# Dense layers in 512-token tiles, more unused products in the gap ahead of the experts, and one low half moved behind an expert's evictions

## What is computed

```python
y = attention_with_decaying_state(r, k, v, w, u)      # B=2, H=8, S=768, head_dim 48
x = y.reshape(1536, 384)
# mixture of 8 experts, one per token, capacity 384 per expert
logits = x @ w_gate; e = argmax(logits); g = softmax(logits)[e]
x = g * (relu(x @ w1[e]) @ w2[e])                     # w1: 384x1024, w2: 1024x384
# dense layers
h = x @ w_in                                          # 384 x 2048
out = (h - tanh(h)) @ w_out                           # 2048 x 384
```

## Time and profile before

| | us |
|---|---|
| median of 3 runs | 419.5 |
| the three runs | 415.28, 419.5, 419.82 |
| the profiled execution | 416.17 |
| its span, first to last instruction | 414.4 |
| TensorE busy | 392.7 (95%) |
| mean granted TensorE clock | 0.966 |

### The profile page before, as it was taken

One profiled execution on the slowest core, in us unless ns is written; L12 is line 12 of the kernel. 1 busy time (PEld: TensorE's weight loads), 2 busy tenths in 40 slices (PEclk: granted clock), 3 DMA queues, 4 the chain that ended last, 5 costly groups with the idle time before them and its releaser, 6 DMA issues.

```text
span 414.4 us, 10465 instructions
## 1 busy us (share of the span) xinstructions
PE 392.7 (95%) x3736; PEld 380.8 (92%) x3737; DVE 211.5 (51%) x453; ACT 182.5 (44%) x486; POOL 155.2 (37%) x132
## 2 busy tenths in 40 slices
PE   5999898999999999999999899999999999999991
PEld 4787777989999999999999899999999999999991
DVE  6365888655556455465455556524343434334340
ACT  5354456432666656657566354533132312231220
POOL 3564676604888815427246043352001100020002
PEclk9999999558999999999999999999999999999997
DMA  7488987443678585685776725101000100010001
GB/s 249 137 253 264 270 247 215 134 153 119 202 241 253 190 269 172 229 262 175 244 232 204 229 69 182 56 1 57 0 0 3 54 0 0 0 57 0 0 1 63
DMA packets 48454, 56.85 MB, mean 137 GB/s; under 512 B 3585, under 2 KB 46017, under 8 KB 48417
## 3 DMA queue, kind: packets, MB, share of 16 engines
q1 hardware_dynamic: 35936, 46.23, 35.5%
q10 hardware_dynamic: 10512, 5.31, 4.5%
q0 software_dynamic: 1968, 4.83, 3.1%
HBM read 46.23 MB, written 10.13 MB: 136 GB/s over the span
## 4 chain that ended last, share of the span: by engine, by line
PE 89%; DVE 5%; issue 2%; DMA 1%; ACT 1%; POOL 0%; POOLq 0%; SPq 0%; DVEq 0%; ACTq 0%
PE ring L1065 13%; PE ring L1067 13%; PE ring L1066 13%; PE pO L1317 8%; PE pO L1316 8%; PE pO L1065 5%; PE pO L1067 5%; PE pO L1066 5%; PE pY L1189 3%; PE pA L1140 2%; PE pD L1094 2%; PE ring L1205 2%; PE pY L1174 1%; PE ring L1254 1%; DVE kw L784 1%
## 5 line engine op out<-in xcount | busy, mean ns | idle before, releaser
L459 POOL TENSOR_TENSOR w_lo<-raw_weights,w_hi 128x768 fp32r<-128x768 f32 x40 | 73.7, 1845 | 85.1 <-ACT w_hi L580 84.9
L1007 DVE SCALAR_TENSOR_TENSOR minus_tanh<-square,ring 128x384 f32<-128x384 f32 x64 | 35.5, 554 | 93.3 <-ACT square L730 93.3
L580 ACT ACTIVATE w_hi<-raw_weights 128x768 fp32r<-128x768 f32 x80 | 67.1, 846 | 24.3 <-DMA raw_weights<-w 24.2
L730 ACT ACTIVATE square<-ring 128x384 f32<-128x384 f32 x64 | 31.5, 491 | 94.3 <-DVE h_hi L1017 53.8
L1065 PE MATMUL ring<-yT_hi,w_hi 128*128 x192 | 65.0, 338 | 1.7 <-DVEq L1002 1.7
L1067 PE MATMUL ring<-yT_hi,w_lo 128*128 x192 | 64.9, 338 | 0.0
L1316 PE MATMUL pO<-w_hi,h_hi 128*128 128x384 f32 x192 | 64.9, 338 | 0.0
L1317 PE MATMUL pO<-w_lo,h_hi 128*128 128x384 f32 x192 | 64.8, 338 | 0.0
L1066 PE MATMUL ring<-yT_lo,w_hi 128*128 x192 | 64.8, 338 | 0.0
L1065 PE MATMUL pO<-h_hi,w_hi 128*128 128x224 f32 x192 | 53.3, 278 | 0.0
L550 POOL DMA_INDIRECT out<-out_rows,tok x12 | 11.7, 974 | 111.1 <-ACT out_rows L725 107.2
(11 more groups left out here) (158 smaller groups left out, 762.3 us busy)
## 6 DMA issues: line engine op xcount, KB each, us to landing
raw_weights<-w SPq DMA_DIRECT2D x80, 384.0 KB, 4.0
x_by_slot<-x ACTq DMA_DIRECT2D x9, 576.0 KB, 5.8
x_expert<-x_by_slot SPq DMA_DIRECT2D x8, 576.0 KB, 5.6
kv<-kv_by_token SPq DMA_DIRECT2D x22, 192.0 KB, 4.3
rkT<-rk_by_feature SPq DMA_DIRECT2D x18, 192.0 KB, 3.8
rkT<-rk_by_feature SPq DMA_DIRECT2D x3, 512.0 KB, 5.3
x_expert<-x_by_slot SPq DMA_DIRECT2D x1, 384.0 KB, 3.0
x_by_slot<-x,sloti POOLq DMA_INDIRECT x12, 4.6
```

The source lines that it names most:

```text
L459: pool.tensor_tensor(lo, unit_raw(2, k), hi.bitcast(F32), ALU.subtract).then_inc(w2_ready, 1)
L580: act.activation(hi, unit_raw(what, k), ACT.Copy).then_inc(w1_hi if what == 1 else w2_hi, 1)
L730: act.activation(sq[:, i % 2, :], ring[i % 4][:, 0:CAP], ACT.Square, scale=THIRD ** 0.5, accum_out=sqsum[:, bass.ds(t * (2 * FC) + i, 1)]) ...
L1007: dve.scalar_tensor_tensor(out=nt[:, i % 2, :], in0=sq[:, i % 2, :], scalar=1.0, in1=ring[i % 4][:, 0:CAP], op0=ALU.subtract, op1=ALU.mult ...
```

## The change

Three things, and what they need of memory:

1. The dense layers go in three tiles of `TD` = 512 tokens instead of four of 384. `ring`'s matmuls stream 512 columns, the second layer has four blocks k and so four banks `pO`. The fourth takes the bank of `pF`; the flag's product goes to `ring[0]`. `ost` has more rows and takes the room of `xTh` and `xTl`, which the dense layers do not need.
2. In the gap, `keep_warm(3)` is new ahead of the last `logits`, `keep_warm(2)` becomes `keep_warm(8)`, and the six products `direct(10)` and `direct(11)` go ahead of the wait for `xe_in` and of `loaded`. `ring_full` is now signalled by `loaded`.
3. On VectorE, `low(e + 1, 3)` goes from ahead of `second` to behind it.

```diff
+TD = 4 * P
+TN = N // TD
...
+        exp = ExitStack()
+        xTh = sb("xT_hi", [P, KD, CAP], F32R, exp)
+        xTl = sb("xT_lo", [P, KD, CAP], F32R, exp)
+        exp.close()
+        ost = sb("out_rows", [P, 2 * KD, D], F32)
+        hh = sb("h_hi", [P, FC, TD], F32R)
...
-        pO = [ctx.enter_context(nc.psum_tensor(f"pO{i}", [P, 512], F32)) for i in range(3)]
-        pF = ctx.enter_context(nc.psum_tensor("pF", [P, 512], F32))
+        pO = [ctx.enter_context(nc.psum_tensor(f"pO{i}", [P, 512], F32)) for i in range(TD // P)]
...
-                    for k in range(4):
+                    for k in range(3):
                         low(e + 1, k, 1 - s)
                     by_width(dve, own, lambda cols: second(j, s, cols))
+                    low(e + 1, 3, 1 - s)
...
             near, far = slice(0, NARROW), slice(NARROW, CAP)
+            keep_warm(3, ones[:, :], pA[:, 0, 0, :])
             logits(STEPS - 1)
...
             direct(9, 2, near, False, False)
-            keep_warm(2, ones[:, :], pX[:, 0:P])
+            keep_warm(8, ones[:, :], pX[:, 0:P])
+            for c in range(KD):
+                direct(10, c, near, False, False)
+                direct(11, c, near, False, False)
             pe.wait_ge(xe_in, 16)
             for c in range(KD):
                 loaded(c, 0, slice(0, P))
-                loaded(c, 1, slice(0, NARROW - P))
-            for c in range(KD):
-                direct(10, c, near, False, False)
-                direct(11, c, near, False, True).then_inc(ring_full, 1)
+                loaded(c, 1, slice(0, NARROW - P)).then_inc(ring_full, 1)
...
+                width = CAP if general else TD
+                blocks = width // P
+                y = bass.ds(t * width, width)
...
-                            last = split_product(ring[i % 4][:, 0:CAP], W1h[:, s, c, f * P:(f + 1) * P],
+                            last = split_product(ring[i % 4][:, 0:width], W1h[:, s, c, f * P:(f + 1) * P],
...
-                    order = [(f, k) for f in range(streamed) for k in range(3)]
-                    order += [(f, k) for k in range(3) for f in range(streamed, FC)]
+                    order = [(f, k) for f in range(streamed) for k in range(blocks)]
+                    order += [(f, k) for k in range(blocks) for f in range(streamed, FC)]
...
-            with pe.Fori(0, TC) as t:
-                dense(t, E * RING + KD, ring_full, ring_done, o_full, o_done, False)
+            with pe.Fori(0, TN) as t:
+                dense(t, E * RING + KD, ring_full, ring_done, o_full, False)
             pe.wait_ge(flag_in, 1)
-            pe.matmul(pF[:, 0:1], ones[:, :], allok[:, :], start=True, stop=True).then_inc(flag_full, 1)
+            pe.matmul(ring[0][:, 0:1], ones[:, :], allok[:, :], start=True, stop=True).then_inc(flag_full, 1)
```

More of the change, by code:

```diff
@@ L261, in build @@
         o_done = sem("o_done")
-        o_sc = [sem(f"o_scattered{i}") for i in range(3)]
+        o_sc = [sem(f"o_scattered{i}") for i in range(TD // P)]
         tok3_made = sem("tok3_made")
@@ L543, in rows_out @@
             def rows_out(done, scattered, t, made):
-                pool.tensor_copy(tok3[:, :], tok_i[:, bass.ds(t * 3, 3)]).then_inc(made, 1)
+                m = len(scattered)
+                pool.tensor_copy(tok3[:, 0:m], tok_i[:, bass.ds(t * m, m)]).then_inc(made, 1)
                 pool.wait_ge(made, t + 1)
-                for i in range(3):
-                    pool.wait_ge(done, t * 3 + (i + 1))
+                for i in range(m):
+                    pool.wait_ge(done, t * m + (i + 1))
                     pool.sem_inc(passed, 1)
@@ L554, in landed @@
             def landed(scattered, t):
-                for i in range(3):
+                for i in range(len(scattered)):
                     pool.wait_ge(scattered[i], t * 16 + 16)
-            with pool.Fori(0, TC - 1) as t:
+            with pool.Fori(0, TN - 1) as t:
                 rows_out(o_done, o_sc, t, tok3_made)
@@ L718, in _, with rows @@
                     by_width(act, own, lambda cols: second(j, s, cols))
-            def rows(full, done, free, t):
-                for i in range(3):
-                    act.wait_ge(full, t * 3 + (i + 1))
+            def rows(full, done, free, t, m):
+                for i in range(m):
+                    act.wait_ge(full, t * m + (i + 1))
                     if i == 0:
@@ L739, in _ @@
                         high(1, E + 1, k, 1)
-            rows(o_full, o_done, ost_free, 0)
-            with act.Fori(1, TC) as t:
+            rows(o_full, o_done, ost_free, 0, TD // P)
+            with act.Fori(1, TN) as t:
                 for i in range(2 * FC):
                     squares(t, i)
-                rows(o_full, o_done, ost_free, t)
+                rows(o_full, o_done, ost_free, t, TD // P)
             act.wait_ge(flag_ready, 1)
@@ L748, in _ @@
             with act.If(large > 0):
-                for i in range(3):
-                    act.wait_ge(o_sc[i], TC * 16)
+                for i in range(TD // P):
+                    act.wait_ge(o_sc[i], TN * 16)
                 with act.Fori(0, TC) as t:
@@ L1210, in loaded @@
                 at = slice(k * P + cols.start, k * P + cols.stop)
-                pe.matmul(ring[c][:, at], xe[:, k, c * P:(c + 1) * P], ident[:, cols], start=False, stop=False,
-                          skip_group_check=True)
+                return pe.matmul(ring[c][:, at], xe[:, k, c * P:(c + 1) * P], ident[:, cols], start=False, stop=True,
+                                 skip_group_check=True)
             near, far = slice(0, NARROW), slice(NARROW, CAP)
+            keep_warm(3, ones[:, :], pA[:, 0, 0, :])
             logits(STEPS - 1)
@@ L1295, in _, with dense @@
                     by_width(pe, own, lambda cols: second(j, s, cols))
-            def dense(t, base, full, done, o_full, o_done, general):
-                y = bass.ds(t * CAP, CAP)
+            def dense(t, base, full, done, o_full, general):
+                width = CAP if general else TD
+                blocks = width // P
+                y = bass.ds(t * width, width)
                 for s in range(2):
@@ L1347, in _ @@
                 with pe.Fori(0, TC) as t:
-                    dense(t, 0, g_ring_full, g_ring_done, g_o_full, g_o_done, True)
+                    dense(t, 0, g_ring_full, g_ring_done, g_o_full, True)
 def kernel(r, k, v, w, u, moe_w_gate, moe_w1, moe_w2, moe_capacity, moe2_w_in, moe2_w_out):
```

49 lines of the change are left out of this document (22 added, 27 removed).

## The result

| | before | changed |
|---|---|---|
| median of 4 runs, us | 417.39 (415.22 to 419.82) | 421.81 (418.95 to 424.26) |
| the profiled execution, us | 416.17 | 421.67 |
| its span, us | 414.4 | 419.8 |
| mean granted clock in it | 0.966 | 0.962 |

The ratio is 1.019, with a 95% interval of 1.012 to 1.026: in this measurement, of four executions each, the changed kernel was 1.9% slower. The forecast was 419.1 us and no difference; 421.8 lies just outside its range.

A forecast was written before the change was run, and what follows sets the result against it. The prediction took TensorE as the bound: matmul count, spacing, its few stands, and half clock in the gap. Terms -2.9 (tiles) + 0.9 (low half) + 1.6 (gap) = -0.4 us gave 419.1 us on the median; range 413.0 to 421.5.

The forecast's parts named there:

- From there on TensorE never stands up to 98.65: Gap: after three unused products push `logits` by 0.62 us, all later work moves by 0.62; whole gap term +1.6 us.
- Rival E: Gap: the fill costs more than the dense layers give, up to +3.2 us; total +1.2, time 420.7; chance 0.24.
- rise at 95.85: Gap: the clock rises from half speed at 95.85 as in the trace before, giving the +1.6 us term.
- rival B: Gap: the fill lifts the clock early, gap term 0; total -2.0 us, time 417.5; chance 0.14.
- 512 columns, -2.9 us: Dense layers: 432 `ring` matmuls at 228 ns, 98.5 us, replace 576 at 176 ns, 101.4 us; -2.9 us.
- The line through two widths: Dense layers: a straight line through 224 columns (111 ns) and 384 (176 ns) gives 228 ns for 512.
- rival C: Dense layers: time on top of the columns vanishes, 213.3 ns per matmul, -9.2 us; total -6.7, time 412.8; chance 0.05.
- The moved low half, +0.9 us: End of the last expert: the low half delays the signal TensorE awaits before the dense layers; +0.9 us, bounds 0 and +1.0.
- the same 0.96 us stands between the evictions and the signal: Last expert, VectorE: the moved low half's 0.96 us comes before signal `y_ready`, for which TensorE waits; taken as +0.9 us.
- The lower bound, 0: End of the last expert: least cost allowed for the moved low half, 0 against the +0.9 us taken.
- The base: Whole kernel: difference set against 419.5 us, median of three timed runs; the profiled execution took 416.17 us.
- the bound of 0 for the 512-column matmuls: Dense layers: keeping the 384-column rate per column, 234.7 ns per matmul, the wider tiles gain exactly 0.

The follow-up runs named there:

- p3_gap_back: Kernel before plus fill and reorder, with nine products taken out of a body not entered, so later code is unmoved; ratio 1.001, median 0.0 us against before.
- e1_tiles: Kernel before with the 512-token dense tiles alone, gap and VectorE's order as before; ratio 0.998, median -0.9 us against before.
- p2_after_back: Changed kernel with nine products taken out of a body not entered, moving later code back; ratio 0.996, median -3.5 us against before.
- f2_no_fill: Changed kernel without the nine additional unused products; tiles, reorder and moved low half stay; ratio 0.995, median -2.6 us against before.
- e2_gap: Kernel before with the gap's part alone, nine more unused products and the reorder; ratio 1.007, median +5.9 us against before.
- g2_no_fill_pad: f2_no_fill plus nine unused products in a body not entered, so later code moves; ratio 1.012, median +4.7 us against before.
- f3_pad4: Kernel before with four unused products in a body not entered, so only later code moves; ratio 0.999, median +3.0 us against before.
- f1_changed: The changed kernel run again on another chip, with twelve executions; ratio 0.999, median +3.3 us against before.
- p1_pad: Kernel before with nine unused products in a body not entered, so only later code moves; ratio 1.012, median +5.2 us against before.

## Why the prediction was wrong

**The sum left out the code itself.** For part 2 I counted each added product's time and each wait, and "From there on TensorE never stands up to 98.65" was carried on to the first expert: the 0.28 us of "issue" at 100.06 was taken as a constant. This step failed: it is the end of a jump, it was 0.28 to 1.41 us in kernels with unmoved code, and it became 1.75 to 3.5 us in the kernels with the code moved by nine products, with a second stand of 1.5 to 2.6 us in the second expert in all of them but the first profile of the changed kernel (there the transfer had landed at 127.34, ahead of the transposes at 128.27, while in the other four it began behind their start; why it came early is open). The prediction had no term for where the code stands, and no rival with one.

Rival E had the right sign and the right place, but its price was the fill's execution. That price is there, but hardly counts. p3_gap_back and e1_tiles both spend 3.4 us of the gap at half clock. From the start of the last `logits` to the last unused products it is 96.40 - 85.27 = 11.13 us with the fill, and 93.02 - 83.24 = 9.78 without, so the fill takes TensorE 1.35 us in this pair of profiles. But the first expert's matmul comes 12.63 and 12.26 us behind `logits`, only 0.37 us apart, since e1_tiles then stands 1.34 us and p3_gap_back 0.36. In the whole kernel the fill's execution is lost in the noise: p3_gap_back is at 0.0 us by the median, with a ratio interval worth -1.8 to +2.8 us, and p2_after_back against f2_no_fill, on two chips, is at -3.5 and -2.6.

**The clock.** I let it rise at 95.85 as in the trace of before. In the changed kernel's profile it was up by 92, as rival B had it, but kernels with the old gap had it up by then too (in e1_tiles four MATMUL of unused products take 0.45 us at 88.6, which is full speed), so nothing shows that the fill did that. There is a hint: in the five profiles with the fill the clock rose 4.2 to 6.0 us behind the start of the last `logits`, in the twelve without it 4.4 to 10.3 us, five of them over 8. The profile that I took the sum from, with 10.3, was the latest of all. What I did not price is the clock after a stand: half for some 3.4 us behind the first expert's stand, about 1.5 us, in all five kernels moved by nine products. At the start of the dense layers it fell in the changed kernel and e2_gap, and not in e1_tiles or f2_no_fill, with the same 1.7 to 1.8 us stand; what decides that stays open.

**512 columns, -2.9 us.** Measured 233.3 ns in the changed kernel, from these starts of one half tile of 72 matmuls (16.80 us):

```profile
298.70 0.40 PE L1069 MATMUL ring<-yT_hi,w_hi 128*128 x1
...
315.50 0.34 PE L1323 MATMUL pO<-w_hi,h_hi 128*128 128x384 f32 x1
```

and 229.0 in e1_tiles (16.49 us):

```profile
287.60 0.39 PE L1068 MATMUL ring<-yT_hi,w_hi 128*128 x1
...
304.09 0.34 PE L1321 MATMUL pO<-w_hi,h_hi 128*128 128x384 f32 x1
```

So 432 of them are 100.8 or 98.9 us against 101.4, a gain of 0.6 or 2.5 us. The line through two widths was right within 0.5% for one of these and 2.3% for the other. Of eight profiles six have 233 and two (e1_tiles, g2_no_fill_pad) 229, each for all its tiles; what sets it stays open. Nothing near rival C's 213 occurred.

**The moved low half, +0.9 us.** Wrong: the stand grew from 1.72 to 1.82 us, and even that is not clear of chance, since p3_gap_back and f3_pad4, in which no low half has moved, have 1.81 and 1.84. VectorE's timeline there in the changed kernel, with TensorE's start:

```profile
239.32 1.08 DVE L979 TENSOR_TENSOR yT_lo<-pO,yT_hi 128x224 f32 x3 [2.79 <-ACT yT_hi L709]
240.31 0.95 DVE L852 TENSOR_TENSOR w_lo<-raw_weights,w_hi 128x768 fp32r<-128x768 f32 x1
241.20 0.58 PE L1069 MATMUL ring<-yT_hi,w_hi 128*128 x1 [1.82 <-DVEq L1006]
```

The low half runs to 241.26, and TensorE starts at 241.20: the signal did not wait for it. The step that failed is "the same 0.96 us stands between the evictions and the signal"; VectorE's sequencer went through its branches and the signal while the low half ran. That is read from these times, as the signal itself has no row here. The lower bound, 0, was the answer.

**The base.** The median of 419.5 was of three runs; a fourth made it 417.39, and 35 executions on another chip had 412.4. A difference set against a median of three carried some 2 us of chance, and here the chance was kind: a forecast of -0.4 us on 417.39 would have been 417.0, missed by 4.8 us and not by 2.7.

**The range.** It was narrower than its own terms. With the bound of 0 for the 512-column matmuls, which the prediction gives itself, rival E comes to 0 + 0.9 + 3.2 = +4.1 us, or 423.6; and rival C's 412.8 lies below the range's 413.0. A measured 421.8 inside a wider range would have been right by luck, since none of the terms held the stand on code.

## What to carry to other kernels

An edit that adds instructions moves every instruction behind it. A jump whose target has slid out of the fetched blocks showed here as a stand of 1.5 to 3.5 us, at two places; with the half clock behind it, nine products in a body that is not entered cost 5 us by the median in one pair of kernels and 7 in another. Before an unused product or an unrolled body goes in ahead of a branch, look at the engine's "issue" time behind that branch, and measure the same edit once with as many instructions taken out of (or put into) a body that is not entered: it tells the work from its place. In a kernel whose executions spread by 2.5%, four of each are too few for a part worth half a per cent: with twelve, the intervals here are still 0.3 to 0.6% to either side.

## What was not expected of the hardware

- A stand on instructions is put down to "issue" or, falsely, to the last semaphore event of another engine (xT_lo, which ended 0.03 to 0.83 us ahead of the matmul in e2_gap, f1_changed and p1_pad). The steady sign was the distance from a queue-8 transfer's landing, 1.55 to 1.70 us at the first place in five kernels and 1.3 to 1.4 us at the second in four; with unmoved code the first matmul came at most 0.45 us behind the landing.
- The signal behind a VectorE operation can reach TensorE while that operation still runs (241.20 against 241.26).
- The same matmul of 512 columns starts every 229.0 or every 233.3 ns, one value throughout an execution.
